# Splitting the turned x on VectorE straight out of the accumulator, in a kernel of a seven-tap mixing and two feed-forward nets

## The reference

```
w   = softmax(weight_gen, over 7 taps)         # 8 heads of 24 channels
x   = sum_k w[k] * x_in[token - 6 + k]         # zeros ahead of each batch
xn  = x / sqrt(mean(x*x) + 1e-6) * rms_g
y   = (silu(xn @ w_gate) * (xn @ w_val)) @ w_out1      # d_ff 1536
out = gelu_sigmoid(y @ w_in) @ w_out2                  # d_ff 2048
```

## Time and profile before

| | us |
|---|---|
| median of 3 runs | 1229.71 (1229.64 to 1229.87) |
| the profiled execution | 1229.53 |
| its span, first to last instruction | 1227.6 |
| PE busy | 1218.5 (99%) |
| PEld busy | 1120.0 (91%) |
| DVE busy | 775.9 (63%) |
| ACT busy | 681.0 (55%) |
| POOL busy | 59.9 (5%) |

### The profile page before, as it was taken

One profiled execution on the slowest core, in us unless ns is written; L12 is line 12 of the kernel. 1 busy time (PEld: TensorE's weight loads), 2 busy tenths in 40 slices (PEclk: granted clock), 3 DMA queues, 4 the chain that ended last, 5 costly groups with the idle time before them and its releaser, 6 DMA issues.

```text
span 1227.6 us, 28952 instructions
## 1 busy us (share of the span) xinstructions
PE 1218.5 (99%) x12025; PEld 1120.0 (91%) x12025; DVE 775.9 (63%) x1203; ACT 681.0 (55%) x1222; POOL 59.9 (5%) x65
## 2 busy tenths in 40 slices
PE   8999999999999999999999999999999999999998
PEld 6879999899999988989989999999989989999998
DVE  8887574856749566484764848557485664944533
ACT  5656655455564655646565454655545556464554
POOL 5323000000000000000000000000000000000000
PEclk9999999999999999999999999999999999999999
DMA  7220010100101001010010001001010000000000
GB/s 206 85 69 30 18 33 2 50 2 18 33 5 47 1 18 34 17 34 2 18 33 18 33 2 39 13 18 34 5 47 1 18 33 2 14 1 15 1 15 14
DMA packets 15456, 33.09 MB, mean 27 GB/s; under 512 B 1892, under 2 KB 8804, under 8 KB 15328
## 3 DMA queue, kind: packets, MB, share of 16 engines
q1 hardware_dynamic: 15328, 31.26, 7.9%
HBM read 24.96 MB, written 6.29 MB: 25 GB/s over the span
## 4 chain that ended last, share of the span: by engine, by line
PE 97%; DVE 2%; issue 0%; ACT 0%; DMA 0%; POOL 0%; DVEq 0%; ACTq 0%
PE up_ps L979 48%; PE acc L979 36%; PE acc L983 6%; PE up_ps L983 6%; DVE h_lo L940 0%; PE acc L1244 0%; DMA logits<-in_weight_gen_dram 0%; DVE mixed_eps L781 0%; DVE tap L777 0%; PE acc L1245 0%; DVE probs L723 0%; DVE hidden L929 0%; ACT L637 0%; ACT h_hi L661 0%; PE acc L1252 0%
## 5 line engine op out<-in xcount | busy, mean ns | idle before, releaser
L940 DVE TENSOR_TENSOR h_lo<-hidden,h_hi 128x512 fp32r<-128x512 f32 x448 | 313.9, 701 | 353.8 <-ACT h_hi L661 352.5
L661 ACT CAST h_hi<-hidden 128x512 fp32r<-128x512 f32 x448 | 278.1, 621 | 247.1 <-DVE hidden L929 234.8
L979 PE MATMUL acc<-out_w,h_hi 64*128 64x384 f32 x1024 | 302.0, 355 | 0.0
L983 PE MATMUL acc<-out_w,h_hi 64*128 64x384 f32 x1024 | 301.9, 355 | 0.0
L654 ACT ACTIVATE hidden<-up_ps 128x512 f32<-128x512 f32 x256 | 152.7, 596 | 189.8 <-PE up_ps L983 189.6
L979 PE MATMUL acc<-out_w,h_lo 64*128 64x192 f32 x1024 | 253.1, 247 | 0.0
L983 PE MATMUL acc<-out_w,h_lo 64*128 64x192 f32 x1024 | 253.0, 247 | 0.0
L979 PE MATMUL up_ps<-x_hi,up_w 64*128 64x512 f32 x752 | 236.7, 394 | 0.0
L983 PE MATMUL up_ps<-x_hi,up_w 64*128 64x512 f32 x752 | 234.7, 392 | 0.0
L979 PE MATMUL acc<-h_hi,out_w 64*128 64x512 f32 x576 | 195.5, 393 | 2.4 <-DVE y_f L876 1.3
L983 PE MATMUL acc<-h_hi,out_w 64*128 64x512 f32 x576 | 195.2, 392 | 0.0
(11 more groups left out here) (145 smaller groups left out, 3193.7 us busy)
## 6 DMA issues: line engine op xcount, KB each, us to landing
x_win<-in_x_dram SPq DMA_DIRECT2D x14, 960.0 KB
out_dram<-out_sb SPq DMA_DIRECT2D x15, 384.0 KB, 2.3
stage<-in_moe_w_out_dram SPq DMA_DIRECT2D x13, 192.0 KB, 3.0
logits<-in_weight_gen_dram SPq DMA_DIRECT2D x16, 112.0 KB, 2.0
stage<-in_moe_w_in_dram SPq DMA_DIRECT2D x4, 256.0 KB, 3.1
stage<-in_moe_w_gate_dram SPq DMA_DIRECT2D x3, 256.0 KB, 4.8
stage<-in_moe_w_gate_dram SPq DMA_DIRECT2D x5, 128.0 KB, 4.4
stage<-in_moe_w_val_dram SPq DMA_DIRECT2D x5, 128.0 KB, 4.6
```

The lines of the kernel that those rows point to most:

```text
L661: nc.scalar.copy(h_hi[:, u % 4, :], hidden[:, u % 2, :]).then_inc(hi_ready, 1)
L940: nc.vector.tensor_tensor(h_lo[:, u % 4, :], hidden[:, u % 2, :], h_hi[:, u % 4, :].bitcast(F32), ALU.subtract).then_inc(lo_ready, 1)
L979: return nc.tensor.matmul(ps, w[TOP], data[TOP], start=start, stop=stop)
L983: return nc.tensor.matmul(ps, w[LOW], data[LOW], start=start, stop=stop)
```

## The change

In blocks 1 to 14 ScalarE no longer reads `turned`: `scale_main` and its `scale_rest` at unit 11 are dropped (a `scale_rest` for group 1 in block 0 stays). VectorE reads it: after the `h_lo` of unit 11 `split_turned` scales and rounds `turned` to `x_hi` in one instruction, and makes `x_lo` in two, one for each bank, out of `turned` and `x_hi`; after the `h_lo` of unit 12 VectorE runs `scale_rest`, two instructions. At unit 17 only `split_rest` is left. On TensorE visit 0 of the first `down2` waits for `x_ready` (both halves of `x_lo` written) in place of `x_scaled`, and no longer for `out_ready`, a count that was reached long before. Visit 1 waited for `main_out` and `rest_out` ahead of its first matmul; now the top matmul waits for `main_out` alone, and the low one behind it for `rest_out`.

```diff
 # scalar: def scale_main(g), removed
-                act.wait_ge(x_turned, g + 1)
-                act.wait_ge(x_ready, g * 2)
-                nc.scalar.activation(x_f32[:, 0, :].rearrange("p (j h c) -> p j h c", j=STEP, h=2),
-                                     turned[:, :, 0:2 * P].rearrange("p h (j c) -> p j h c", j=STEP),
-                                     ACT.Copy, scale=g_main[:, :]).then_inc(x_scaled, 1)
 # scalar: run
-                    elif i and mixing and u == X_T:
-                        scale_main(i + 1)
-                        scale_rest(i + 1)
 # vector
-            def split_x(g):
-                dve.wait_ge(up_done, unit_at(g - 1, U1))
-                dve.wait_ge(x_scaled, g - 1)
-                split_main(g, x_f32, x_hi, x_lo, x_hi_ready, x_ready)
+            def halves(data):
+                return [data.rearrange("p (j h c) -> p h j c", j=STEP, h=2)[:, h] for h in range(2)]
+
+            def split_turned(g):
+                dve.wait_ge(x_turned, g + 1)
+                dve.wait_ge(up_done, unit_at(g - 1, U1))
+                src = [turned[:, h, 0:2 * P].rearrange("p (j c) -> p j c", j=STEP) for h in range(2)]
+                nc.vector.tensor_scalar_mul(x_hi[:, :].rearrange("p (j h c) -> p j h c", j=STEP, h=2),
+                                            turned[:, :, 0:2 * P].rearrange("p h (j c) -> p j h c", j=STEP),
+                                            g_main[:, :]).then_inc(x_hi_ready, 1)
+                dve.wait_ge(x_hi_ready, g + 1)
+                for h in range(2):
+                    ins = nc.vector.scalar_tensor_tensor(halves(x_lo[:, :])[h], src[h], g_main[:, :],
+                                                         halves(x_hi[:, :].bitcast(F32))[h], ALU.mult, ALU.subtract)
+                ins.then_inc(x_ready, 1)
+
+            def scale_rest(g):
+                to = x_f32[0:REST, 1, :].rearrange("p (a b h c) -> p a b h c", a=2, b=2, h=2)
+                for b in range(2):
+                    part = slice(b * REST, (b + 1) * REST)
+                    ins = nc.vector.tensor_scalar_mul(
+                        to[:, :, b, :, :], turned[part, :, 2 * P:3 * P].rearrange("p h (a c) -> p a h c", a=2),
+                        g_rest[part, :])
+                ins.then_inc(rest_scaled, 1)
+
+            def split_x_rest(g):
                 dve.wait_ge(rest_scaled, g + 1)
                 split_rest(g, x_f32, x_rest, x_twin, rest_hi, x_ready)
 # vector: run, after the h_lo of unit u
+                    if i and mixing and u == U1 - 1:
+                        split_turned(i + 1)
+                    if i and mixing and u == U1:
+                        scale_rest(i + 1)
                     if i and mixing and u == SPLIT_X:
-                        split_x(i + 1)
+                        split_x_rest(i + 1)
 # tensor: down2(i, p), p == 0, i < GROUPS; v is the visit
                     elif i < GROUPS and v == 0:
-                        pe.wait_ge(x_scaled, min(i, GROUPS - 2))
+                        pe.wait_ge(x_ready, 2 * min(i + 1, GROUPS - 1) + 1)
                         pe.wait_ge(rest_scaled, min(i + 2, GROUPS))
-                        if i > 1:
-                            pe.wait_ge(out_ready, i * 2 - 2)
                     elif i < GROUPS:
                         pe.wait_ge(main_out, i + 1)
-                        pe.wait_ge(rest_out, i + 1)
 # tensor: the same, for each of the visit's two units n
                         top(acc[:, at_top, 0:2 * D], h[:, t], w, start=first)
+                        if first and v == 1 and i < GROUPS and p == 0:
+                            pe.wait_ge(rest_out, i + 1)
                         low(acc[:, at_low, 0:2 * D], h[:, q], w, start=first)
```

More of the change, by code:

```diff
@@ L272, in mix_and_two_ffns @@
         exps, squared, rstd, main_normed = (sem(n) for n in ("exps", "squared", "rstd", "main_normed"))
-        x_turned, x_scaled, x_hi_ready, x_ready = sem("x_turned"), sem("x_scaled"), sem("x_hi_ready"), sem("x_ready")
+        x_turned, x_hi_ready, x_ready = sem("x_turned"), sem("x_hi_ready"), sem("x_ready")
         main_turned, twin_ready = sem("main_turned"), sem("twin_ready")
@@ L576, in round_main @@
                                      ACT.Copy, scale=g_main[:, :]).then_inc(x_hi_ready, 1)
-            def scale_main(g):
-                act.wait_ge(x_turned, g + 1)
-                act.wait_ge(x_ready, g * 2)
-                nc.scalar.activation(x_f32[:, 0, :].rearrange("p (j h c) -> p j h c", j=STEP, h=2),
-                                     turned[:, :, 0:2 * P].rearrange("p h (j c) -> p j h c", j=STEP),
-                                     ACT.Copy, scale=g_main[:, :]).then_inc(x_scaled, 1)
             def scale_rest(g):
```

## The result

Over 12 runs each, the kernel before took 1229.74 us and the changed one 1226.77 us (1226.60 to 1227.14). The ratio is 0.9975, with a 95% interval of 0.9967 to 0.9984. That is 2.97 us less where 2.66 were forecast, right at the fast edge of the range, 1226.7. The profiled execution took 1227.05 us.

The account below looks back on a forecast made before the run. TensorE, busy nearly throughout, was taken to bound the kernel, stalling at visit 1 for `rest_out`. Saving 0.19 us in each of 14 blocks gave 2.66 us: 1229.71 to 1227.05, stated as 1227.1 us, range 1226.7 to 1228.9.

Parts of the forecast that it names:

- What bounds it, and which semaphore: First `down2`, blocks 1 to 14: TensorE waits 0.14 us at visit 1, plus some 0.05 us restart, for `rest_out`.
- ScalarE's part: Unit 11: without the copies of `turned`, the first GELU starts 1.94 us after `h_hi` instead of 3.36.
- The rival built on the Trainium skill's 2.66 us for load and drain: ScalarE after unit 11: first GELU no earlier, at 1079.53, visit 1 loses another 0.2 us a block; 1232.5 us, chance 0.06.
- VectorE's part: Units 11 to 13: added `x_hi` 0.69 us, `x_lo` and `scale_rest` halves 0.48 each, hidden with 0.75 us left.
- The sum of the first steps: First to second `down2`: 4.38 us in blocks 1 to 14, saving 0.19 us a block, 2.66 us in all.
- Unit 17: VectorE at unit 17: `x_hi` and `x_lo` leave it, they stood in slack, so nothing gained.
- rival 4: Rest of each block: other distances shrink too, beyond the stall; 1226.5 us at the most, chance 0.02.
- by itself would gain next to nothing: Visit 1, low matmul's separate wait for `rest_out`: a few hundredths of a us more room, alone next to no gain.

## Why the prediction was right or wrong

**What bounds it, and which semaphore** was right. The page's waits didn't show the stall; the distances did. Two copies on ScalarE, or three instructions on VectorE, bring it back from either engine, and the rest of x scaled on ScalarE shows that it is a threshold.

**ScalarE's part** was right: the GELU came 1.93 us behind `h_hi`, forecast 1.94. The table load took 1.28 us and the GELU followed 1.29 us after its start. The rival built on the Trainium skill's 2.66 us for load and drain ("ScalarE: Activation LUTs", "What ACT_TABLE_LOAD costs") didn't come about.

**VectorE's part** was right in its order and nearly so in its size: `x_hi` took 0.74 us, a little more than the 0.69 taken, the halves of `x_lo` and of the rest 0.48 each as taken; 0.78 us were left idle (0.75 reckoned). One more instruction of 0.74 us cost nothing.

**The sum of the first steps** was right: 4.38 us in each (4.41 in block 2), and 2.62 us saved in the 14 of them, forecast 2.66.

**The step that failed** is "Unit 17": "They stood in VectorE's slack and nobody waits for them before the next block: nothing". Nobody waits for `x_hi` and `x_lo`, but in block 1 `h_lo` is queued behind them, and GpSimd slows them to where this matters. So the term put at nothing was worth about 0.24 us, shown from both sides: later in the kernel before it goes away (4.56 to 4.38 us), put back in the changed one it returns (4.38 to 4.54). The same oversight is in rival 4, "Other distances in the block shrink too": it got a chance of 0.02 because "the rest of the block fits block 15's", and that holds for block 14 but not for block 1, where two more steps did shrink. I had compared one steady block as a whole, and of block 1 only the first step, and multiplied by 14. The sign was in the rows shown: L809's mean of 498 ns in the earlier trace rows stands over the 420 ns that it takes in all blocks but one; in block 1 it takes 1516. By the Trainium skill's "SBUF — State Buffer", section "SBUF: two separate sides", a VectorE instruction in a two-port mode, or one with two SBUF inputs beside a GpSimd instruction that reads SBUF, shares a port pair with GpSimd; whoever starts first holds it for the whole instruction. The trace agrees in kind: the cast ends 0.29 us after GpSimd's instruction, where one that starts only then would end 0.42 us after it (the ends of GpSimd's spans are rough). It agrees the other way round too: GpSimd's subtraction of 128x384 takes 1.41 us where an `h_lo` has started just ahead of it (114.77 against 114.92), and the same form just before, with VectorE idle, 1.02.

**A second step was wrong without moving the number:** that the waits taken apart "by itself would gain next to nothing". By itself it gains 1.48 us. I had left out that a wait in front of a matmul holds its weight load too, and that a half that once lags doesn't pay for the same lag in each block again. In the full change there is nothing left for it to gain (1226.66 us with the waits together).

The remaining 0.07 us between 2.90 and 2.97 is within what the runs scatter.

## What to carry to other kernels

On an engine that is 99% busy, read distances between starts in a block that has the suspected cause and in one that lacks it; the list of waits may show nothing. Before multiplying one block's saving by all blocks, look at the slowest instance of each instruction that moves, not at its mean, and at what GpSimd does beside it. If two parts of a change cure the same lateness, one may be enough: with the copies gone from ScalarE, taking the waits apart added nothing; and with the waits apart, leaving ScalarE its 64-channel copies gave the same time as taking all copies away. Whether moving the 128-channel copy alone is enough with the waits together, no run shows.

## What the runs showed of the hardware

A wait placed ahead of a matmul holds back its weight load too: in the kernel before, both loads of visit 1 start at the release (1084.29 and 1084.33), 0.33 us after the load before them, where around them one load follows another within 0.2 us. The upper and lower 64 rows can run 0.14 to 0.18 us apart from block to block, and a standing lag takes up a later wait: 0.09 us instead of 0.19 a block. The lag costs about its own length once, when both halves are held together (6.96 us with a lag of 0.17 and 6.79 with none, on the way into block 16). VectorE's cast of 128x512 in SBUF took 0.42 us alone and 1.5 us beside GpSimd's subtractions of 1.6 us.
